# One feature half of the logits moved ahead of the last transposes, the column softmax cut in three pieces, and its denominators computed during the slot sums

## The reference, cut to what matters

```python
logits = x @ phi                                   # 3072 x 32
d = np.exp(logits - logits.max(0, keepdims=True))  # column softmax, over the tokens
d /= d.sum(0, keepdims=True) + 1e-09
slot_input = d.T @ x                               # 32 slots x 320
...                                                # h = relu(slot_input[e] @ w1[e]); slot_out[e] = h @ w2[e]
c = np.exp(logits - logits.max(1, keepdims=True))  # row softmax, over the slots
c /= c.sum(1, keepdims=True) + 1e-09
x2 = c @ slot_out
out = ((x2 @ w_a) * (x2 @ w_b)) @ w_out
```

## Time and profile before

| | |
|---|---|
| median of three runs | 274.70 us (274.69 to 275.26) |
| the profiled execution | 274.15 us, of it 272.4 us span of the core |
| granted TensorE clock, mean of the core | 1.00 |
| PE busy | 244.9 us (90% of the span) |
| DVE busy | 181.3 us (67%) |
| ACT busy | 88.2 us (32%) |
| POOL busy | 65.3 us (24%) |

### The profile page before, as it was taken

How to read it: one execution, slowest core, us unless ns; L and a number is a source line. 1 busy time by engine, 2 the same in 40 slices (tenths; PEclk the granted TensorE clock), 3 DMA queues, 4 the chain that set the end, 5 groups by cost and what they waited for, 6 DMA issues and landing times.

```text
span 272.4 us, 7971 instructions
## 1 busy us (share of the span) xinstructions
PE 244.9 (90%) x3264; PEld 204.4 (75%) x3264; DVE 181.3 (67%) x458; ACT 88.2 (32%) x145; POOL 65.3 (24%) x100
## 2 busy tenths in 40 slices
PE   0459889789897999999899998999999999999995
PEld 0448889778786898989569626665767779999995
DVE  6981778768685868787558506347998866544550
ACT  3659511122222231322333005432900023444431
POOL 9422152414141334257501304320000000000000
PEclk9999999999999999999999999999999999999999
DMA  6967999999899776610899999970000001222222
GB/s 228 361 168 262 267 220 264 278 281 284 254 298 262 214 215 179 191 28 2 327 411 427 423 424 439 431 310 0 2 0 0 2 0 67 77 99 75 93 91 82
DMA packets 22436, 54.73 MB, mean 201 GB/s; under 512 B 4000, under 2 KB 14400, under 8 KB 21248
## 3 DMA queue, kind: packets, MB, share of 16 engines
q1 hardware_dynamic: 18320, 50.24, 54.5%
q10 hardware_dynamic: 4080, 3.98, 5.8%
HBM read 49.99 MB, written 4.23 MB: 199 GB/s over the span
## 4 chain that ended last, share of the span: by engine, by line
PE 69%; DVE 13%; ACT 5%; DMA 5%; issue 3%; SPq 2%; POOL 1%; ACTq 1%; DVEq 0%; POOLq 0%
PE ps L988 59%; PE ps L1204 4%; DVE attn L754 4%; DMA attn<-kk 4%; PE ps L1079 3%; ACT xreg L577 2%; DVE attn L766 1%; SPq L442 1%; DVE attn L767 1%; DVE xreg L780 1%; POOL xTreg L486 1%; PE ps L1085 1%; DMA xTreg<-ig 1%; PE ps L1210 1%; DVE attn L737 1%
## 5 line engine op out<-in xcount | busy, mean ns | idle before, releaser
L988 PE MATMUL ps<-attn 128*64 128x41 f32 (+3 forms) x2016 | 88.9, 247 | 8.0 <-issue 3.3
L988 PEld LDWEIGHTS ps<-attn 128*64 128x64 f32 (+1 forms) x2016 | 82.6, 135 | 15.7 <-issue 7.2
L508 POOL TENSOR_TENSOR attn<-attn 128x160 f32<-128x160 f32 x48 | 21.1, 461 | 73.1 <-issue 51.5
L754 DVE SCALAR_TENSOR_TENSOR attn<-attn,small,ps 128x41 f32<-128x41 f32 x176 | 30.9, 248 | 4.5 <-PE ps L988 4.5
L988 PE MATMUL ps<-Whr,Phr 128*128 128x320 f32 x96 | 30.0, 313 | 0.0
L988 PE MATMUL ps<-Whr,Plr 128*128 128x320 f32 x96 | 29.7, 309 | 0.0
L988 PE MATMUL ps<-Wlr,Phr 128*128 128x320 f32 x96 | 29.7, 309 | 0.0
L592 ACT COPY xTreg<-ps 128x512 f32<-128x512 f32 x22 | 12.7, 587 | 52.2 <-PE ps L1079 52.2
L988 PE MATMUL ps<-woreg,tlow 128*128 128x320 f32 x96 | 26.3, 433 | 0.0
L988 PEld LDWEIGHTS ps<-woreg,tlow 128*128 128x128 f32 x96 | 18.1, 190 | 7.8 <-issue 0.5
L957 DVE TENSOR_TENSOR Plr<-tail,Phr 128x512 fp32r<-128x512 f32 x20 | 13.8, 691 | 13.0 <-ACT Phr L663 13.0
(11 more groups left out here) (165 smaller groups left out, 342.0 us busy)
## 6 DMA issues: line engine op xcount, KB each, us to landing
attn<-kk SPq DMA_DIRECT2D x24, 416.0 KB, 7.4
front<-w SPq DMA_DIRECT2D x10, 512.0 KB, 9.2
tail<-w SPq DMA_DIRECT2D x10, 512.0 KB, 7.8
xTreg<-w SPq DMA_DIRECT2D x4, 1280.0 KB, 14.0
xreg<-og SPq DMA_DIRECT2D x4, 960.0 KB, 7.9
xreg<-w SPq DMA_DIRECT2D x3, 1280.0 KB, 12.1
front<-wab SPq DMA_DIRECT2D x1, 3840.0 KB, 15.8
out<-tlow SPq DMA_DIRECT2D x24, 160.0 KB, 1.8
```

Source lines behind the costliest of these rows:

```text
L508: last = g.tensor_tensor(ksb[n % 2][:, c, 0:HU * D].rearrange("r (h e) -> r h e", h=HU), knb[n % 3][:, c], last_col[:, c].unsqueeze(2).to_ ...
L754: last = v.scalar_tensor_tensor(out=C[:, cc + 1, p], in0=C[:, cc, p], scalar=dcy[:, 2 * u + p, cc:cc + 1], in1=pUv[:, p, c, 0:VW], op0=ALU ...
L988: return t_.matmul(o_, l_, r_, start=start, stop=stop)
```

## The change

PE: `logits(half, g)` issues eight matmuls. The two calls for `g = 0` now stand before and after the last transpose group `turn(23)`, the two for `g = 1` follow; the six filler transposes before the logits are gone. Banks: logits go to `ps[2]` and `ps[3]` in place of `ps[0]` and `ps[1]`, and other small results move to free banks. ACT: the exponential is three instructions of 512 columns; each writes one bank's worth of `dT` doubled by a repeated read of `Lsb`, with a sum of its own; ACT's three `dz` copies now stand ahead of the row exponential. DVE: after `negmax` it waits for all three pieces, adds their sums, makes `seld` (times 0.5, as every value is counted twice), copies its halves of `dz`, and only then does the row maxima, the subtraction and `rec`. PE: the transposes wait for one piece at a time; the denominator matmul stands ahead of the slot sums; the filler count before the transposes goes from 17 to 3.

```diff
-GAP_LOGITS, GAP_MAX, GAP_EXP, GAP_PART, GAP_SLOTS = 6, 9, 17, 3, 8
+GAP_MAX, GAP_EXP, GAP_PART, GAP_SLOTS = 9, 3, 3, 8
...
-            for a_ in range(2):
-                s.activation(dT[:, :, a_], Lsb.rearrange("r (c t) -> r c t", c=NC), ACT.Exp, bias=negmax,
-                             accum_out=dsum[a_]).then_inc(one["d_sb"], 1)
-            act.wait_ge(one["lsub_sb"], 1)
-            s.activation(Ed[:, :, 0:32], Ed[:, :, 0:32], ACT.Exp).then_inc(one["e_tok"], 1)
+            for i in range(3):
+                s.activation(dT[:, 4 * i:4 * i + 4], Lsb[:, 256 * i:256 * i + 256].rearrange("r (c t) -> r c t", c=4).unsqueeze(2).to_broadcast([128, 4, 2, L]),
+                             ACT.Exp, bias=negmax, accum_out=dsum[:, i:i + 1]).then_inc(one["d_sb"], 1)
             act.wait_ge(one["dz_zero"], 1)
             for i in range(3):
                 act.wait_ge(one["d_t"], i + 1)
                 s.copy(dz[0:64, 4 * i:4 * i + 4, :, 0:SLOTS], dt_ps(i)[0:64]).then_inc(one["dz_a"], 1)
+            act.wait_ge(one["lsub_sb"], 1)
+            s.activation(Ed[:, :, 0:32], Ed[:, :, 0:32], ACT.Exp).then_inc(one["e_tok"], 1)
...
-            v.tensor_copy(negmax, ps[3][:, 0:1]).then_inc(one["negmax_sb"], 1)
+            v.tensor_copy(negmax, ps[1][:, 0:1]).then_inc(one["negmax_sb"], 1)
+
+            v_.wait_ge(one["d_sb"], 3)
+            chain(v.reduce_sum(dtot, dsum, AX_X))
+            v.tensor_scalar(seld, cs[:, C_SEL:C_SEL + SLOTS], dtot, 0.5, ALU.mult, ALU.mult).then_inc(one["seld_sb"], 1)
+            v_.wait_ge(one["dz_zero"], 1)
+            for i in range(3):
+                v_.wait_ge(one["d_t"], i + 1)
+                v.tensor_copy(dz[64:128, 4 * i:4 * i + 4, :, SLOTS:2 * SLOTS], dt_ps(i)[64:128]).then_inc(one["dz_v"], 1)
...
-            v_.wait_ge(one["d_sb"], 1)
-            v.tensor_scalar(seld, cs[:, C_SEL:C_SEL + SLOTS], dsum[0], None, ALU.mult).then_inc(one["seld_sb"], 1)
-            v_.wait_ge(one["dz_zero"], 1)
-            for i in range(3):
-                v_.wait_ge(one["d_t"], i + 1)
-                v.tensor_copy(dz[64:128, 4 * i:4 * i + 4, :, SLOTS:2 * SLOTS], dt_ps(i)[64:128]).then_inc(one["dz_v"], 1)
+            v_.wait_ge(one["den_ps"], 1)
+            chain(v.tensor_scalar(rec, ps[1][:, 32:64], 1e-9, None, ALU.add))
+            chain(v.reciprocal(rec, rec))
...
-            chain(v.tensor_scalar(rec, ps[3][:, 96:128], 1e-9, None, ALU.add))
-            chain(v.reciprocal(rec, rec))
...
-            for m in range(NB - 6, NB):
+            for m in range(NB - 6, NB - 1):
                 turn(m)
-
-
             pe.wait_ge(w_sb, NB)
-            keep_clock(ps[3], GAP_LOGITS)
+            pe.wait_ge(ld_phi, 16)
+            pe.wait_ge(xT_sb, NB - 3)
+            logits(0, 0)
+            turn(NB - 1)
+            logits(1, 0)
             pe.wait_ge(xT_sb, NB - 2)
             pe.wait_ge(xT_sv, 2)
-            pe.wait_ge(ld_phi, 16)
-            pe.wait_ge(e_sb, NB)
             for half in range(2):
-                for i in range(4):
...
+                logits(half, 1).then_inc(one["logits_ps"], 1)
...
-            keep_clock(ps[1], GAP_EXP)
-            pe.wait_ge(one["d_sb"], 2)
+            keep_clock(ps[3], GAP_EXP)
             for c in range(NC):
+                if c % 4 == 0:
+                    pe.wait_ge(one["d_sb"], c // 4 + 1)
...
+            pe.wait_ge(one["seld_sb"], 1)
+            mm(ps[1][:, 32:64], ones, seld).then_inc(one["den_ps"], 1)
```

More of the change, by code:

```diff
@@ L159, in build @@
         o += NT * 64
-        colmax, negmax, *dsum = (small[:, o + i:o + i + 1] for i in range(4))
+        colmax, negmax, dtot = (small[:, o + i:o + i + 1] for i in range(3))
+        dsum = small[:, o + 4:o + 7]
         rmax = small[:, o + 8:o + 8 + NT]
@@ L282, in build @@
         one = {n: sem(n) for n in (
-            "logits_ps", "half_max", "logits_sb", "colmax_sb", "colmax_t", "maxrow_sb", "negmax_ps", "negmax_sb", "d_sb", "d_t",
+            "logits_ps", "half_max", "den_ps", "logits_sb", "colmax_sb", "colmax_t", "maxrow_sb", "negmax_ps", "negmax_sb", "d_sb", "d_t",
             "dz_zero", "p4_zero", "w4_zero", "dz_a", "dz_v", "ltok_ps", "lsub_sb", "e_tok", "ed_ready", "slot_ps", "part_sb", "seld_sb",
@@ L609, in _ @@
                 act.wait_ge(one["half_max"], half + 1)
-                s.copy(Lsb[:, 384 * half:384 * half + 384], ps[half][:, 0:384]).then_inc(one["logits_sb"], 1)
+                s.copy(Lsb[:, 384 * half:384 * half + 384], ps[2 + half][:, 0:384]).then_inc(one["logits_sb"], 1)
             act.wait_ge(one["negmax_sb"], 1)
             act.wait_ge(one["logits_sb"], 2)
-            for a_ in range(2):
-                s.activation(dT[:, :, a_], Lsb.rearrange("r (c t) -> r c t", c=NC), ACT.Exp, bias=negmax,
-                             accum_out=dsum[a_]).then_inc(one["d_sb"], 1)
-            act.wait_ge(one["lsub_sb"], 1)
-            s.activation(Ed[:, :, 0:32], Ed[:, :, 0:32], ACT.Exp).then_inc(one["e_tok"], 1)
+            for i in range(3):
+                s.activation(dT[:, 4 * i:4 * i + 4], Lsb[:, 256 * i:256 * i + 256].rearrange("r (c t) -> r c t", c=4).unsqueeze(2).to_broadcast([128, 4, 2, L]),
+                             ACT.Exp, bias=negmax, accum_out=dsum[:, i:i + 1]).then_inc(one["d_sb"], 1)
             act.wait_ge(one["dz_zero"], 1)
@@ L825, in _ @@
                 v_.wait_ge(one["logits_ps"], half + 1)
-                v.reduce_max(colmax2[:, half:half + 1], ps[half][:, 0:384], AX_X).then_inc(one["half_max"], 1)
+                v.reduce_max(colmax2[:, half:half + 1], ps[2 + half][:, 0:384], AX_X).then_inc(one["half_max"], 1)
             v_.wait_ge(one["half_max"], 2)
@@ L829, in _ @@
             v_.wait_ge(one["colmax_t"], 1)
-            chain(v.reduce_max(maxrow, ps[2][0:1, 0:128].rearrange("r (b s) -> r s b", b=B), AX_X))
+            chain(v.reduce_max(maxrow, ps[0][0:1, 0:128].rearrange("r (b s) -> r s b", b=B), AX_X))
             v.tensor_scalar(nmrow.rearrange("r (b s) -> r b s", b=B), maxrow.unsqueeze(1).to_broadcast([1, B, SLOTS]),
@@ L1113, in _, with logits @@
                     turn(n - 6)
-            for m in range(NB - 6, NB):
+            def logits(half, g):
+                for hp in range(2):
+                    for b in range(B):
+                        last = mm(ps[2 + half][32 * b:32 * b + 32, 0:384].rearrange("r (c t) -> r c t", c=6), phis[:, g, hp],
+                                  xT[:, g, b, 6 * half:6 * half + 6, hp * L:hp * L + L], start=(g == 0 and hp == 0), stop=(g == 1 and hp == 1))
+                return last
+            for m in range(NB - 6, NB - 1):
                 turn(m)
             pe.wait_ge(w_sb, NB)
-            keep_clock(ps[3], GAP_LOGITS)
+            pe.wait_ge(ld_phi, 16)
[3 more added lines that the diff above has]
+            logits(1, 0)
             pe.wait_ge(xT_sb, NB - 2)
             pe.wait_ge(xT_sv, 2)
-            pe.wait_ge(ld_phi, 16)
-            pe.wait_ge(e_sb, NB)
             for half in range(2):
-                for i in range(4):
[L1126 to L1131, removed]
+                logits(half, 1).then_inc(one["logits_ps"], 1)
+            keep_clock(ps[1], GAP_MAX)
             pe.wait_ge(one["colmax_sb"], 1)
-            t_.transpose(ps[2][0:1, 0:128], colmax, ident).then_inc(one["colmax_t"], 1)
+            t_.transpose(ps[0][0:1, 0:128], colmax, ident).then_inc(one["colmax_t"], 1)
             pe.wait_ge(one["logits_sb"], 2)
@@ L1159, in _ @@
             last.then_inc(one["slot_ps"], 1)
-            keep_clock(ps[1], GAP_PART)
+            keep_clock(ps[7], GAP_PART)
             pe.wait_ge(one["part_sb"], 1)
@@ L1170, in _ @@
             for j in range(4):
-                mm(ps[3][32 * j:32 * j + 32, 64:96], part[:, 128:160], selh(j % 2))
-            mm(ps[3][:, 96:128], ones, seld).then_inc(one["sT_ps"], 1)
-            keep_clock(ps[1], GAP_SLOTS)
+                last = mm(ps[3][32 * j:32 * j + 32, 64:96], part[:, 128:160], selh(j % 2))
+            last.then_inc(one["sT_ps"], 1)
+            keep_clock(ps[7], GAP_SLOTS)
             pe.wait_ge(one["sT_sb"], 1)
```

2 lines of the change are left out of this document (1 added, 1 removed).

## The result

The changed kernel took 279.75 us (median, 278.65 to 280.71), against 274.98 for the kernel before in the same comparison (274.69 to 275.44): a ratio of 1.0163, 95% interval 1.0119 to 1.0208. It is slower: by 4.8 us between the two medians, by 4.5 us between the profiled executions (278.65 against 274.15 us, with spans of 276.9 and 272.4). Two of the four executions, 278.65 and 279.07 us, had a mean granted clock of 0.994, the other two, 280.43 and 280.71 us, one of 0.986 and 0.987, which is about twice as long at the lower clock. Only the first was profiled, so where the last two lost their time isn't shown.

What follows compares the result with a forecast made beforehand. The chain from logits through exponential and slot sums to the hidden layer's start was taken as bounding; DVE's later list +0.65 and held casts +2.38 gave +3.03 us on 274.15, so 277.2, or 277.7 on the median; range 274.8 to 279.8.

Steps and rivals of the forecast that it cites:

- the clock's case: PE idle from about 150.7 to 155.7 us: casts held and TensorE's clock falls, 279.7 to 280.7 us; chance 0.15.
- The likeliest case: DVE's casts held by POOL's clearing, clock stays: 277.7 us, own range 276.8 to 278.5; chance 0.36.
- Logits: PE around the last transpose group: logits end at 137.25 instead of 138.72 us, a gain of about 1.45 us.
- Exponential: ACT's three pieces at 0.75 us each; DVE's first `dz` copy 1.41 us earlier, all from the logits.
- DVE behind it: Row maxima and subtraction, 2.07 us, come behind the `dz` copies; DVE reaches `part` at 153.01, 1.31 us later.
- The casts: DVE's two casts beside POOL's clearing of `P4r`: held between 0 and 2.38 us, the upper bound taken.
- not held: DVE's casts run unhindered beside POOL's clearing: +0.65 us, 275.35 us, own range 274.9 to 276.0; chance 0.35.
- From `part` to the hidden layer: PE's eight fillers end later than the multiplications: 2.15 us, hidden layer starts at 155.16 against 154.51, +0.65 us.

Runs made afterwards that it cites:

- the late clearing: The changed kernel with POOL's clearing of `P4r` waiting for the copy `part` instead of the slot sums: 277.65 us, ratio 1.0101.

## Why the prediction held, step by step

The direction was right. That the range held the time is in part luck: the median of 279.75 lies 0.05 us inside the upper bound of 279.8, and two of the four executions lie above it. I had called that bound one that takes in most of the clock's case, but I had priced that case at 279.7 to 280.7, so it took in only the lower end. The likeliest case did not come: I gave 277.7 for casts held with the clock unharmed (0.36), and what came was the rival of casts held and clock fallen (279.7, which I had given 0.15). All steps below are counted from the last transposes.

*Logits.* Forecast 1.45 us; they ended 137.55 - 129.06 = 8.49 behind the last transposes' start, before 138.72 - 128.85 = 9.87: 1.38, and alone 1.35 in the stretch. Right.

*Exponential.* Pieces 0.72 apart (0.75 forecast); DVE's first `dz` copy 13.82 behind the start, before 15.23: 1.41 earlier, as forecast. That the pieces bring nothing is shown by the kernel with two pieces and 17 fillers (0.05 us), in the order with the maxima in front; there too DVE waits for all pieces before its copies. In the changed order itself it was not tried. What I missed is that shorter pieces also shorten a gap of PE, which the 17 fillers had been there to cover.

*DVE behind it.* Forecast: `part` 1.31 us later without the hold. It came 155.37 - 129.06 = 26.31 behind the start, before 22.85, so 3.46 later, of which the casts are 2.85 - 0.63 = 2.22 and the rest 1.24. The kernel with the maxima in front shows that this order is the cause of the whole loss: putting it right removes the late list, the overlap with the clearing and the long idle time at once, 6.2 us. That is more than the 4.31 lost, because what the change gains then shows: 1.35 at the logits, and 33.10 - 32.61 = 0.49 in the kernel with two pieces and 17 fillers against the logits alone. The 0.49 are those of the denominators and `rec` together with the small moves beside them; no run has these alone.

*The casts.* The upper bound of 2.38 was right, 2.22 measured; the late clearing brings them back to 0.64. For "held" I had only one tensor_scalar. The trace of the kernel before had two held casts that I overlooked, from float32 to bf16, beside POOL instructions that read and write SBUF:

```profile
9.97 2.31 POOL L486 TENSOR_TENSOR xTreg<-xTreg 32x768 f32<-32x768 f32 x1 [2.86 <-ACT xTreg L581]
13.22 1.95 POOL L486 TENSOR_TENSOR xTreg<-xTreg 32x768 bf16<-32x768 f32 x1 [0.94 <-ACT xTreg L584]
```

```profile
10.82 1.88 DVE L708 CAST xTreg<-xTreg 32x768 bf16<-32x768 f32 x1
13.71 1.88 DVE L710 CAST xTreg<-xTreg 32x768 bf16<-32x768 f32 x1
...
16.50 0.54 DVE L342 CAST attn<-small 82x768 bf16<-82x768 f32 x1
```

Each of the two ends 0.42 us behind POOL's instruction, and a cast of as many columns took 0.54 with POOL idle. These rows leave open whether a memset, which reads nothing, does the same, but they speak against the 0.35 that I gave to "not held".

The Trainium skill (SBUF — State Buffer, section Who interferes with whom) has it that a 2-port DVE instruction and a GpSimd instruction exclude each other whole; the traces agree, for a POOL instruction that only writes too (2592 ns in place of 341), and with the clearing in eight pieces the wait is by instruction (1061 and 646 ns).

*From `part` to the hidden layer.* Forecast 2.15 (the terms as written add up to 2.17); it was 156.25 - 154.03 = 2.22 in the kernel with late clearing and 20 fillers, at full clock, and 158.58 - 155.37 = 3.21 in the changed kernel. The difference of 0.99 is the clock, and so is 9.24 - 8.72 = 0.52 in the hidden layer: 1.5 together, as filling the idle time gave back 1.48. The step that went wrong is a chance: I held "no row shows a fall after fast work" against the rival and gave the fall 3 chances in 10 once the casts were held. Its price, 2 us, was put half a microsecond too high for the profiled execution; the late clearing shows one of nearly 3 (1.33, 1.90 and 10.28 against 0.83, 1.02 and 8.72 us: 2.94).

*The not-held case* was forecast at +0.65 and measured at +0.59 in the stretch by taking hold and clock away.

## What to carry to other kernels

When a wait is moved forward in an engine's list, look at the work that used to run while it would now be waiting, and at how much slack the last instruction of that list had: here 2.07 us of work went behind a wait, against a slack of 0.36 us. Then ask what the late list runs beside that it did not meet before (here POOL's clearing), and which engine idles meanwhile (here PE). The late list by itself cost 35.05 - 32.56 = 2.49 us, which the gains of the change brought down to 0.6; the two consequences, 2.2 us at the casts and 1.5 at the clock, cost more. And fillers ahead of a gap belong to the gap: when the work around them is moved, they have to be counted again.

## What the runs showed of the hardware

A POOL memset, which reads nothing, holds a DVE cast from SBUF to SBUF until it ends: 2592 ns in place of 341, beside a memset of 2663 ns. DVE instructions with two SBUF sources beside memsets weren't held: 0.56 us at 153.43 in the kernel with eight pieces, whose memsets ran from 151.5 to 154.8 us, as without them, and the earlier trace rows.

TensorE's clock fell from 2.4 to 1.2 GHz around idle times of 4.81, 3.59, 2.59 and 1.75 us in four kernels: half a microsecond before the end of the one of 2.59 us, and 0.3 to 0.7 us behind the end of the others. It did not fall with 1.82 and 1.21 us elsewhere in the same part of the program, nor with 1.49 us in the kernel before. The length of the idle time alone doesn't tell, as the same instructions of the attention at about 57 us show. After 1.94 us without work the clock fell at about 59 us in the profile of the late clearing with 20 fillers; after 1.94 us it stayed in that of two pieces with 3 fillers, and after 2.31 us in that of two pieces with 17. What decides was not found; 20 and 10 fillers in the gap kept the clock in one profile each. In this stretch a fall cost between 1.5 and 2.9 us.

One full-width matmul of 32 columns in float32 among the half-width slot sums lengthened them from 6.74 to 7.23 us (146.17 + 4.57 less 143.51). Behind them it ran while PE would have waited for `part`, and the stretch was 0.49 us shorter.
